# The second tile's matrix scaled and turned in the middle of VectorE's inverse of the first tile

## The chip, the cores and the metric

The kernel runs on one core of one Trainium2 chip. The metric is the time of one execution on the device, in microseconds (us), as the median of several runs.

## The reference

Two parts follow each other. The first is a delta rule over 768 positions, for 4 batches and 8 heads with 48 dimensions; its output, 3072 tokens of 384 values, goes through two feed-forward layers with 2048 hidden values each. Only the first part is touched by the change:

```python
k_n = k / (norm(k) + 1e-06)
for t in range(S):
    y[:, :, t] = einsum('bhd,bhde->bhe', q[:, :, t], state)
    v_old = einsum('bhde,bhd->bhe', state, k_n[:, :, t])
    state = state + beta[t] * einsum('bhd,bhe->bhde', k_n[:, :, t], v[:, :, t] - v_old)
# y: (tokens, 384); then h = x @ w_in, a function of h by element, and g @ w_out, twice
```

## The kernel before, in words

The positions are cut into chunks of C = 32. Four chunks make a tile, so there are T = 6 tiles of 128 positions. Within a chunk the 32 updates depend on each other through a triangular matrix; its inverse turns the 32 steps into matmuls. Each tile has 4 chunks, 4 batches and 8 heads, 128 such matrices of 32 x 32. For the inverse they lie one on each of the 128 partitions, 1024 elements each.

**The inverse** is made by `rounds` (L204 to L218). It starts from the unit matrix and goes through r = 31 down to 1. Round r is a multiply of r x (32 - r) elements into `inv_t` (L214) and a subtract of the same shape into `inv` (L217), each with a wait for the one before: 62 tensor_tensor instructions for one tile, of 31 to 256 elements per partition. All their inputs and outputs are in SBUF. VectorE does tile 0, and GpSimd does tiles 1 to 5, one behind the other. The arguments `first` and `last` of `rounds` give the range of r, and `done` is the count of the engine's own semaphore that has been reached.

**What an inverse needs.** TensorE multiplies keys with keys and queries of a tile (the Gram matrices, `gram_fill`, L374). VectorE then does, for tile j: `weights(j)` (L618 to L625, four short instructions on the norms and beta), four `scale_gram(j, f)` (L641, L642, two multiplies from PSUM each, into `n_mat` and `p_mat`), and two `turn_n(j, ...)` (L659, transposes of half the matrix each into `n_turned`). The second `turn_n` of a tile releases the inverse of that tile on GpSimd. When an inverse is ready, VectorE turns it back with two `turn_x` (L668) into `x_mat`.

**The order of the work** is written out by hand: each engine has one program, and semaphores tie them. VectorE's begins with tile 0's norms, Gram scaling and turning, then the whole inverse of tile 0, then `turn_x(0)`, `residual(0, 0, 0)` (L678), `spread_w(0)` (L650), and then tile 1's `weights`, `scale_gram` and `turn_n`. Behind that comes the loop over tiles and their 8 steps s (4 chunks c, 2 groups g of heads). In a step VectorE does `updates` (L689, from the solve's result), the `residual` of the next step (L678, from the product of keys and state), and `copy_low` (L695, the state). TensorE does in a step: `solve` (L405), a share of the Gram products of the tile two ahead (L374), `q_state` (L418), the next step's `k_state` (L392), `turn_y` (L461), `update` (L432) and `within` (L446). ScalarE copies and scales. The matrix of tile 2 is turned in step 7 of tile 0, that of tile tau + 2 in steps 3 and 4 of tile tau.

Ahead of each tile TensorE runs `keep_warm(BURST)`, 12 matmuls on a zeroed tile whose result nobody reads (L357). For tile 0 it waits for all 62 instructions of VectorE's inverse (`dve_step`), and behind the burst for all eight Gram fills to be scaled (`gram_used`). For the later tiles it waits for the inverse (`inv_ready`). SP issues the loads, each when TensorE or VectorE has done with what lay there; VectorE issues no DMA.

Of the kernel before, what the change touches and what calls it, by code (L numbers as in the profile page):

```python
# [13 lines left out]
C = 32  # L14
# [104 lines left out]
def delta_rule(nc, kq_t, kv_n, beta_n, consts, x1, w1, w, hand):  # L119

    with ExitStack() as ctx:
# [6 lines left out]
        def sem(name):  # L128
            return ctx.enter_context(nc.semaphore(name))
# [47 lines left out]
        pool_step, dve_step = sem("pool_step"), sem("dve_step")  # L177
# [15 lines left out]
        def index(tau, c, g):  # L193
            return NQ * tau + G2 * c + g
# [12 lines left out]
        def rounds(eng, tt, j, own, step, done, first, last):  # L207

            for r in range(first, last, -1):
                shape = [P, r, C - r]  # L210
                prod = inv_t[:, own, 0:r * (C - r)].rearrange("p (i k) -> p i k", i=r)
                if done:
                    eng.wait_ge(step, done)
                tt(prod, n_turned[:, j % 2, r, 0:r].unsqueeze(2).broadcast_to(shape),  # L214
                   inv[:, j % 2, r:r + 1, r:C].broadcast_to(shape), ALU.mult).then_inc(step, 1)
                eng.wait_ge(step, done + 1)
                tt(inv[:, j % 2, 0:r, r:C], inv[:, j % 2, 0:r, r:C], prod, ALU.subtract).then_inc(step, 1)  # L217
                done += 2  # L218
            eng.wait_ge(step, done)
# [364 lines left out]
        def _(dve):  # L584
            dve_tt = nc.vector.tensor_tensor
# [27 lines left out]
            def weights(j):  # L613

                def done(k):
                    dve.wait_ge(norm_step, NORM_STEPS * j + k)
                done(4)
                nc.vector.tensor_scalar(norm[:, j], scratch[:, 3], 0.5, 1e-6, ALU.mult, ALU.add).then_inc(norm_step, 1)  # L618
                done(5)
                nc.vector.reciprocal(scratch[:, 4], norm[:, j]).then_inc(norm_step, 1)  # L620
                done(6)
                dve_tt(scratch[:, 5], scratch[:, 4], beta[:, j], ALU.mult).then_inc(norm_step, 1)
                done(7)
                dve_tt(wgt[:, j], scratch[:, 5], scratch[:, 4], ALU.mult).then_inc(norm_step, 1)
                done(8)  # L625
# [19 lines left out]
            def spread_w(j):  # L645

                if j >= 2:
                    dve.wait_ge(ublk_ready, NQ * (j - 1))
                shape = [P, CG, B]
                dve_tt(w_blk[:, j % 2], wgt[:, j].unsqueeze(2).broadcast_to(shape),  # L650
                       blk_mask[:].unsqueeze(1).broadcast_to(shape), ALU.mult).then_inc(wblk_ready, 1)

            def turn_n(j, a, b):

                dve.wait_ge(gram_used, 4 * j + 4)
                if j >= 3:

                    dve.wait_ge(inv_ready, j - 2)
                nc.vector.transpose(n_turned[:, j % 2, a:b], n_mat[:].rearrange("p n k -> p k n")[:, a:b]  # L659
                                    ).then_inc(n_turned_ready, 1)  # L660

            def turn_x(j, a, b):

                if j:
                    dve.wait_ge(inv_ready, j)
                if j >= 2:
                    dve.wait_ge(hz_done, NQ * (j - 1))
                nc.vector.transpose(x_mat[:, j % 2].rearrange("p n k -> p k n")[:, a:b],  # L668
                                    inv[:, j % 2].rearrange("p i k -> p k i")[:, a:b]).then_inc(x_ready, 1)

            def residual(tau, c, g):
                q = index(tau, c, g)
                dve.wait_ge(nv_ready, q + 1)
                dve.wait_ge(ks_done, q + 1)

                def split(t):
                    return t.rearrange("p (r v) d -> p r v d", r=HALVES)
                dve_tt(split(z[:, g]), split(kv_run[:, c, 1, U * g:U * g + U]),  # L678
                       ks_ps[:, 0:U * D].rearrange("p (v r d) -> p r v d", v=V, r=HALVES), ALU.subtract).then_inc(z_ready, 1)
# [18 lines left out]
            half_k, half_n = C // 2, CG // 2  # L698
# [11 lines left out]
            turn_n(0, half_k, C)  # L710
            dve.wait_ge(inv_blank, 2)
            dve.wait_ge(n_turned_ready, TURNS)
            rounds(dve, dve_tt, 0, 1, dve_step, 0, C - 1, 0)
            turn_x(0, 0, half_k)
            turn_x(0, half_k, C)
            residual(0, 0, 0)
            spread_w(0)
            weights(1)
            for f in range(4):
                scale_gram(1, f)  # L720
            turn_n(1, 0, half_k)
            turn_n(1, half_k, C)
            split = {(T - 2, 2): 0, (T - 2, 6): 1, (T - 1, 2): 2, (T - 1, 6): 3}
            for tau in range(T):
                for s in range(NQ):
# [482 lines left out]
```

## Time and profile before

| | |
|---|---|
| median of 3 runs | 1130.83 us (1129.53 to 1133.27) |
| the profiled execution, own time | 1131.52 us |
| its span | 1129.7 us |
| mean granted TensorE clock | 0.958 |
| TensorE busy | 1026.9 us (91%) |
| VectorE busy | 870.2 us (77%) |
| ScalarE busy | 779.8 us (69%) |
| GpSimd busy | 227.1 us (20%) |

The profile is of one execution of the program. PE is TensorE's matmuls and PEld its weight loads, DVE is VectorE, ACT ScalarE, POOL GpSimd, SP the queue that issues most of the loads. The span begins with the first instruction, and times in the timeline count from there. In a timeline a line gives start, duration, engine, source line, operation, output and inputs, and in brackets the idle time of the engine ahead of it with what ended it; neighbouring instructions of the same kind are put together, with their count behind an x. The delta rule takes the first 292 us of the span, the feed-forward layers the rest. The granted clock is given in shares of TensorE's full 2.4 GHz.

### The profile page before, as it was taken

The numbers are of one execution on the slowest core, as the hardware profiler recorded it, in microseconds if no ns is written. First come the engines' busy times: TensorE is split into PE (matmuls) and PEld (weight loads), VectorE is DVE, ScalarE is ACT, GpSimd is POOL, SyncE is SP. The second block draws the span as 40 slices with busy tenths as digits, with TensorE's granted clock in tenths as the row PEclk, the third lists the DMA queues.
The fourth block names the chain that finished last, engine by engine and source line by source line (L and its number), as shares of the span: only waits on it lengthen the run. The fifth ranks groups of instructions, "written<-read, shape, count | busy, mean of one in ns | idle before, by whom it ended". The sixth has DMA issues, their size and how long they took to land.

```text
span 1129.7 us, 24251 instructions
## 1 busy us (share of the span) xinstructions
PE 1026.9 (91%) x10280; PEld 816.6 (72%) x10280; DVE 870.2 (77%) x948; ACT 779.8 (69%) x991; POOL 227.1 (20%) x380
## 2 busy tenths in 40 slices
PE   4488888888778999999999997999999999999997
PEld 3266666666667888777787876778888888888885
DVE  5966666565388888897887868999787878888885
ACT  1133444465598999989989987986776767676764
POOL 5087888880000010010010000000000000000000
PEclk7578999899989999999999999999999999999999
DMA  7823443323443333435234363430100001010000
GB/s 178 237 60 101 115 130 101 84 77 101 118 91 77 80 91 73 111 63 123 56 67 116 60 168 85 121 112 1 57 1 23 32 0 56 0 56 1 29 1 28
DMA packets 35104, 86.99 MB, mean 77 GB/s; under 512 B 4416, under 2 KB 12096, under 8 KB 35008
## 3 DMA queue, kind: packets, MB, share of 16 engines
q1 hardware_dynamic: 27584, 59.13, 17.3%
q0 software_dynamic: 6912, 25.17, 11.7%
q10 hardware_dynamic: 512, 1.31, 0.5%
q8 instruction: 73, 1.20, 0.4%
q14 instruction: 23, 0.19, 0.1%
HBM read 46.27 MB, written 14.16 MB: 53 GB/s over the span
## 4 chain that ended last, share of the span: by engine, by line
PE 34%; DVE 20%; ACT 12%; issue 6%; DMA 1%; ACTq 0%; DVEq 0%; POOLq 0%
PE o_ps L874 6%; PE o_ps L875 6%; PE o_ps L876 6%; PE h_ps L874 6%; PE h_ps L876 6%; PE h_ps L875 6%; DVE val L1098 5%; DVE den L1055 5%; ACT rec L962 4%; DVE pa L1061 3%; ACT rec L970 2%; DVE val L1082 2%; ACT pa L938 2%; DMA val<-pa 1%; DVE den L1089 1%
## 5 line engine op out<-in xcount | busy, mean ns | idle before, releaser
L874 PE MATMUL o_ps<-g_hi,w_hi_early 128*128 128x512 f32 x288 | 115.6, 401 | 20.8 <-DVE g_lo L1104 15.4
L951 ACT ACTIVATE g_hi<-val 128x1024 fp32r<-128x1024 f32 x96 | 102.0, 1062 | 41.8 <-DVE val L1098 36.1
L865 POOL DMA_DIRECT2D val<-pa x48 | 41.4, 862 | 424.5 <-DVE pa L1061 424.5
L874 PE MATMUL o_ps<-g_hi,w_hi_late 128*128 128x512 f32 x288 | 114.1, 396 | 10.4 <-DVE g_lo L1104 9.9
L1098 DVE SCALAR_TENSOR_TENSOR val<-den,val 128x1024 f32<-128x1024 f32 x96 | 117.4, 1222 | 5.0
L1082 DVE TENSOR_TENSOR val<-val,rec 128x1024 f32<-128x1024 f32 x96 | 117.0, 1219 | 5.5 <-DMA val<-pa 5.5
L1104 DVE SCALAR_TENSOR_TENSOR g_lo<-val,g_hi 128x1024 fp32r<-128x1024 f32 x96 | 117.7, 1226 | 2.0 <-ACT g_hi L951 2.0
L875 PE MATMUL o_ps<-g_lo,w_hi_early 128*128 128x512 f32 x288 | 113.9, 396 | 0.0
L876 PE MATMUL o_ps<-g_hi,w_lo_early 128*128 128x512 f32 x288 | 113.5, 394 | 0.0
L874 PE MATMUL h_ps<-x_hi,w_hi_early 128*128 128x512 f32 x288 | 112.3, 390 | 0.7 <-DVE x_lo L1108 0.4
L875 PE MATMUL o_ps<-g_lo,w_hi_late 128*128 128x512 f32 x288 | 112.9, 392 | 0.0
L876 PE MATMUL o_ps<-g_hi,w_lo_late 128*128 128x512 f32 x288 | 112.9, 392 | 0.0
L876 PE MATMUL h_ps<-x_hi,w_lo_late 128*128 128x512 f32 x288 | 112.1, 389 | 0.0
L876 PE MATMUL h_ps<-x_hi,w_lo_early 128*128 128x512 f32 x288 | 112.1, 389 | 0.0
L875 PE MATMUL h_ps<-x_lo,w_hi_early 128*128 128x512 f32 x288 | 112.1, 389 | 0.0
L874 PE MATMUL h_ps<-x_hi,w_hi_late 128*128 128x512 f32 x288 | 112.1, 389 | 0.0
L875 PE MATMUL h_ps<-x_lo,w_hi_late 128*128 128x512 f32 x288 | 112.1, 389 | 0.0
L970 ACT ACTIVATE rec<-rec 128x1024 f32<-128x1024 f32 x96 | 101.0, 1052 | 1.5
L945 ACT ACTIVATE den<-h_ps 128x1024 f32<-128x1024 f32 x48 | 49.3, 1027 | 66.1 <-PE h_ps L876 66.1
L1089 DVE SCALAR_TENSOR_TENSOR den<-den,rec 128x1024 f32<-128x1024 f32 x48 | 58.8, 1224 | 42.7 <-ACT rec L970 42.7
L214 POOL TENSOR_TENSOR inv_t<-n_turned,inv 128x31 f32<-128x31 f32 (+15 forms) x155 | 78.0, 503 | 55.8 <-DVE n_turned L659 40.0
L217 POOL TENSOR_TENSOR inv<-inv,inv_t 128x31 f32<-128x31 f32 (+15 forms) x155 | 86.4, 558 | 12.1
(114 smaller groups left out, 2175.4 us busy)
## 6 DMA issues: line engine op xcount, KB each, us to landing
val<-pa POOLq DMA_DIRECT2D x48, 512.0 KB, 4.6
w_raw<-w SPq DMA_DIRECT2D x16, 768.0 KB, 5.1
kv_run<-kv_n SPq DMA_DIRECT2D x24, 384.0 KB, 3.8
x_raw<-x_dram SPq DMA_DIRECT2D x12, 768.0 KB, 5.7
kq<-kq_t SPq DMA_DIRECT2D x44, 192.0 KB, 4.0
x_dram<-stage SPq DMA_DIRECT2D x12, 384.0 KB, 4.3
x_dram<-stage SPq DMA_DIRECT2D x6, 768.0 KB, 4.2
out<-stage SPq DMA_DIRECT2D x5, 768.0 KB, 4.1
```

The source lines that it names most:

```text
L214: tt(prod, n_turned[:, j % 2, r, 0:r].unsqueeze(2).broadcast_to(shape), inv[:, j % 2, r:r + 1, r:C].broadcast_to(shape), ALU.mult).then_in ...
L217: tt(inv[:, j % 2, 0:r, r:C], inv[:, j % 2, 0:r, r:C], prod, ALU.subtract).then_inc(step, 1)
L874: nc.tensor.matmul(dst, hi, rhs_hi, start=first, stop=False)
L875: nc.tensor.matmul(dst, hi, rhs_lo, start=False, stop=False)
L876: return nc.tensor.matmul(dst, lo, rhs_hi, start=False, stop=last)
L951: act_fn(g_hi[:, n % 2], val[:, n % 2], ACT.Copy, scale=-1.0).then_inc(g_hi_ready, 1)
L970: act_fn(rec[:, e], rec[:, e], ACT.Exp, scale=-1.0).then_inc(rec_ready, 1)
L1055: dve_stt(den[:, e], sq[:, e], cf[:, 6:7], den[:, e], ALU.mult, ALU.add).then_inc(q_ready, 1)
L1082: dve_tt(val[:, e], val[:, e], rec[:, e], ALU.mult).then_inc(ratio_ready, 1)
L1089: dve_stt(den[:, e], den[:, e], ONE, rec[:, e], ALU.add, ALU.mult).then_inc(unit_ready, 1)
L1098: dve_stt(val[:, e], den[:, e], 2.0, val[:, e], ALU.subtract, ALU.mult).then_inc(g_ready, 1)
L1104: dve_stt(g_lo[:, e], val[:, e], -1.0, g_hi[:, e].bitcast(F32), ALU.mult, ALU.subtract).then_inc(g_lo_ready, 1)
```

## The change

VectorE's inverse of tile 0 is cut into two calls. The first does the rounds r = 31 to 16. Then come tile 1's weights, scaling and turning, which stood behind `spread_w(0)`. The second call does the rounds 15 to 1, with the semaphore's count going on at C = 32. Then follow `turn_x`, `residual` and `spread_w` of tile 0 as before. Nothing else changes.

```diff
@@ -710,16 +710,17 @@
             turn_n(0, half_k, C)
             dve.wait_ge(inv_blank, 2)
             dve.wait_ge(n_turned_ready, TURNS)
-            rounds(dve, dve_tt, 0, 1, dve_step, 0, C - 1, 0)
-            turn_x(0, 0, half_k)
-            turn_x(0, half_k, C)
-            residual(0, 0, 0)
-            spread_w(0)
+            rounds(dve, dve_tt, 0, 1, dve_step, 0, C - 1, C // 2 - 1)
             weights(1)
             for f in range(4):
                 scale_gram(1, f)
             turn_n(1, 0, half_k)
             turn_n(1, half_k, C)
+            rounds(dve, dve_tt, 0, 1, dve_step, C, C // 2 - 1, 0)
+            turn_x(0, 0, half_k)
+            turn_x(0, half_k, C)
+            residual(0, 0, 0)
+            spread_w(0)
             split = {(T - 2, 2): 0, (T - 2, 6): 1, (T - 1, 2): 2, (T - 1, 6): 3}
             for tau in range(T):
                 for s in range(NQ):
```

## Rows read from the trace of the kernel before

**Rows 1.** Waits, 0 to 330 us: engine, line waited for, total us, times, longest us.

```profile
POOL inv_t L214 <- DVE n_turned L659: 40.0, 1, 40.0
```

**Rows 2.** Timeline of GpSimd, inverse of tile 1, 57 to 95 us.

```profile
57.89 0.23 POOL L214 TENSOR_TENSOR inv_t<-n_turned,inv 128x31 f32<-128x31 f32 x1 [39.98 <-DVE n_turned L659]
58.20 0.27 POOL L217 TENSOR_TENSOR inv<-inv,inv_t 128x31 f32<-128x31 f32 x1
...
74.89 0.68 POOL L217 TENSOR_TENSOR inv<-inv,inv_t 128x255 f32<-128x255 f32 x1
...
94.31 0.25 POOL L217 TENSOR_TENSOR inv<-inv,inv_t 128x31 f32<-128x31 f32 x1
```

**Rows 3.** Timeline of TensorE, 35 to 107 us.

```profile
35.97 1.75 PE L374 MATMUL turn_ps<-kq 48*32 48x64 f32 x57 [2.38 <-issue]
...
49.55 4.44 PE L357 MATMUL side_ps<-idle 128*128 128x512 bf16 x12 [11.03 <-DVE inv L217]
55.98 0.54 PE L405 MATMUL hz_ps<-z,x_mat 32*32 32x48 f32 x32 [1.99 <-DVE p_mat L642]
...
58.63 1.55 PE L432 MATMUL st_bank<-u_blk,kv_run 128*64 128x192 f32 x8 [0.67 <-DVE u_blk L689]
...
61.55 1.93 PE L374 MATMUL side_ps<-kq 48*32 48x64 f32 x64
...
101.48 4.08 PE L357 MATMUL side_ps<-idle 128*128 128x512 bf16 x12 [1.12 <-issue]
...
105.97 1.10 PE L374 MATMUL side_ps<-kq 48*32 48x64 f32 x64
```

**Rows 4.** Timeline of VectorE, inverse of tile 1 turned, 101 to 104 us.

```profile
101.95 2.12 DVE L668 STREAM_TRANSPOSE x_mat<-inv 128x512 f32<-128x512 f32 x2
```

**Rows 5.** Timeline of VectorE, 38 to 50 us: start us, us, engine, line, operation.

```profile
38.23 0.42 DVE L214 TENSOR_TENSOR inv_t<-n_turned,inv 128x255 f32<-128x255 f32 x1
...
48.99 0.19 DVE L214 TENSOR_TENSOR inv_t<-n_turned,inv 128x31 f32<-128x31 f32 x1
49.22 0.19 DVE L217 TENSOR_TENSOR inv<-inv,inv_t 128x31 f32<-128x31 f32 x1
```

**Rows 6.** Timeline of VectorE, 51 to 107 us.

```profile
51.87 0.20 DVE L618 TENSOR_SCALAR norm<-scratch 128x32 f32<-128x32 f32 x1
...
52.94 0.42 DVE L641 TENSOR_TENSOR n_mat<-st_bank,wgt 128x256 f32<-128x256 f32 x1
...
55.72 2.02 DVE L659 STREAM_TRANSPOSE n_turned<-n_mat 128x512 f32<-128x512 f32 x2
57.66 0.92 DVE L689 TENSOR_TENSOR u_blk<-hz_ps,w_blk 128x768 f32<-128x768 f32 x1
...
65.05 0.35 DVE L678 TENSOR_TENSOR z<-kv_run,ks_ps 128x192 f32<-128x192 f32 x1 [1.75 <-PE ks_ps L392]
...
82.36 0.35 DVE L678 TENSOR_TENSOR z<-kv_run,ks_ps 128x192 f32<-128x192 f32 x1 [4.27 <-PE ks_ps L392]
...
106.10 0.96 DVE L689 TENSOR_TENSOR u_blk<-hz_ps,w_blk 128x768 f32<-128x768 f32 x1 [2.03 <-PE hz_ps L405]
```

**Rows 7.** Timelines of GpSimd and VectorE where both work in SBUF, 80 to 240 us.

```profile
80.07 0.60 POOL L214 TENSOR_TENSOR inv_t<-n_turned,inv 128x247 f32<-128x247 f32 x1
...
129.57 0.59 POOL L217 TENSOR_TENSOR inv<-inv,inv_t 128x192 f32<-128x192 f32 x1
...
129.59 0.62 DVE L611 TENSOR_TENSOR scratch<-scratch,root 128x32 f32<-128x32 f32 x1
...
237.22 2.50 POOL L214 TENSOR_TENSOR inv_t<-n_turned,inv 128x247 f32<-128x247 f32 x1
...
237.51 1.74 DVE L100 TENSOR_TENSOR w_lo_early<-w_raw,w_hi_early 128x1536 fp32r<-128x1536 f32 x1
```

**Rows 8.** Stretches: window, us, busy us (instructions) by engine, granted clock, DMA share, GB/s.

```profile
64.00:66.00 2.00, 2.00 (x30) 1.45 (x22) 0.91 (x3) 0.00 (x0) 1.76 (x4) 0.50 0.31 86
106.00:108.00 2.00, 1.54 (x82) 1.24 (x81) 0.96 (x1) 0.00 (x0) 1.76 (x4) 1.00 0.00 0
```

## The prediction

> **What bounds the kernel now.** The page comes first: the change lies in the first part of the span, where TensorE, VectorE and GpSimd all work and where the GpSimd engine has nearly all of its busy time. The chain of waits is no help here, because it reaches back only to the feed-forward layers. So I read the waits of the stage and then the timeline of each engine.
>
> The waits up to 330 us have one large row for the inverse on GpSimd: it stands idle for 40.0 us until the second tile's turned matrix comes from VectorE [rows 1]. That idle time is what the change shortens. What matters is whether anybody waits at the other end, and no row of that view has an engine waiting for a finished inverse. For tile 1 the timeline shows it directly. GpSimd starts at 57.89 and ends at 94.56 [rows 2]. TensorE starts its burst for tile 1 at 101.48 [rows 3], and VectorE turns the inverse at 101.95 [rows 4]. The inverse lies ready 6.9 us before its first user. The inverses of the later tiles can't start earlier through this change, since tile 2's matrix is turned only in the last step of tile 0.
>
> What does set the start of tile 0 is VectorE. It works without a pause from the first inverse to the first update: rounds 15 to 1 of the inverse from 38.23 to 49.41 [rows 5], turning it, the residual and the spread weights to 51.87, tile 1's weights to 52.94, scaling to 55.72, turning to 57.66. There the first update starts [rows 6]. The matmuls that it needs are done at 56.5 [rows 3]. From then on the tile is a chain between TensorE and VectorE with little slack: each later start of the first update moves everything behind it.
>
> **The work that moves.** Weights, scaling and turning for tile 1 take 57.66 - 51.87 = 5.79 us. They go from behind the spread weights into the middle of the inverse. Nothing is added or removed, and no DMA is issued by VectorE. Tile 1's products are in PSUM at 37.72 [rows 3], and the scaling would start near 38.2 + 1.1 = 39.3, so no wait comes in; if those products came later, VectorE would wait there with the rest of its inverse behind it. I cost this at nothing. SP's loads wait on TensorE and for nothing in this block, and they are issued before it ends; they move with the chain.
>
> Work moved within one engine ahead of the same first update would cost nothing if VectorE set both times. It doesn't quite. TensorE starts a burst of 12 warming matmuls when the inverse is done: 49.55, 0.14 us behind it, for 4.44 us [rows 3]. The first solve is queued behind the burst. Today the burst and the solve are covered by the 5.79 us that now leave. For tile 1, which has no such cover, the first update starts 106.10 - 101.48 = 4.62 us after the burst starts, with a burst of 4.08; with 4.44 it is 4.98, so 5.12 us after the inverse's end [rows 3, 6]. Today it is 57.66 - 49.41 = 8.25. The end of the inverse moves by 5.79, the tail shrinks by 3.13: **+2.66 us**.
>
> **The two engines at once.** This is the largest and the least certain term. Today VectorE has the inverse of tile 0 alone. After the change GpSimd starts its rounds at the moment when VectorE goes on with its rounds 15 to 1, and both are tensor_tensor instructions with two inputs in SBUF. The trace shows what happens between such instructions. VectorE's L100, 1.74 us long, stretches a GpSimd multiply of 247 elements from 0.60 to 2.50; the GpSimd instruction ends 0.47 us after VectorE's. The other way round, L611 starts at 129.59 beside a GpSimd instruction that started at 129.57, and takes 0.62 in place of some 0.19; it ends 0.05 after GpSimd's [rows 7]; the 0.19 is that of 31 elements [rows 5]. So they don't overlap: each waits for the one that came first, and has the first 0.14 of its own duration (0.19 less 0.05; 0.60 less 0.47) behind it by then.
>
> Bounds. Below: nothing, if VectorE always gets in first, as L100 did; a gain has no row, as VectorE alone is the fastest case shown. Above: a whole GpSimd instruction in front of each of the 30. Those 30 that run first take 75.57 - 57.89 = 17.68 us, 0.59 each with a pause of 0.08 (58.12 to 58.20), so 0.51 without it [rows 2]; 30 x 0.51 = 15.3 us. What I take: both engines work in pairs that wait for their own last result, with short pauses of 0.04 on VectorE and 0.08 on GpSimd, so whoever is finished finds the other one waiting, and they alternate. GpSimd then holds 0.51 - 0.14 = 0.37 us per turn, of which VectorE hides its own pause and start, 0.04 + 0.14 = 0.18 [rows 5]. Each of the 30 grows by 0.19: **+5.7 us**. It is nearest to the L611 row, which is the one where both started together. The rounds on VectorE then take 11.2 + 5.7 = 16.9 us.
>
> The Trainium skill, "SBUF — State Buffer", section "Who interferes with whom", speaks against this change: a VectorE instruction with two SBUF inputs contends with a GpSimd one that reads SBUF, and the first to issue has the port for its whole instruction while the other fully blocks. On who blocks, the trace agrees (2.50 in place of 0.60); on the length, the rows show 0.14 less than the whole. By the rule read strictly the sum would be +14.6 us, as in the third rival.
>
> GpSimd loses a similar share, but starts some 13.5 us earlier and ends before 90; its cover of 6.9 us grows.
>
> **TensorE's clock.** Behind the burst TensorE now idles from 53.99 to 55.98, and the steps that follow run at the lower clock: the granted clock reads 0.50 in 64:66, which is 1.2 GHz. It reads 1.00 (2.4 GHz) in 106:108, in tile 1, where the solve follows the burst at once [rows 3, 8]. After the change the solve follows the burst at once here too, so I expect the full clock in tile 0's first two steps. The first state update takes 1.55 us at the low clock; the Gram fill behind the second solve takes 1.93 for 64 matmuls, against 1.10 at the full clock. At that ratio the update saves 0.7. Of VectorE's wait of 1.75 us for the keys' product at 65.05 [rows 6] some 1.5 goes. **-2.2 us**. Bounds: 0 if the clock stays low, and -2.4 if the 1.75 goes whole.
>
> **The sum.** 2.66 + 5.7 - 2.2 = +6.2 us. The profiled execution took 1131.52 us with a span of 1129.7, so 1137.7 for one like it. It lies 0.7 above the median of 1130.83, which I take as the base: 1137.0.
>
> **The rivals.**
> 1. The clock stays at 1.2 GHz in the first steps, because TensorE has idled some 12 us longer ahead of the burst. For it: the clock rose only late in today's burst. Against it: tile 1's. 2.66 + 5.7 = +8.4, 1139.2. Chance 0.18.
> 2. VectorE hardly waits, because its next instruction takes the port before GpSimd's: as with L100, where GpSimd had started 0.29 earlier and still waited. Against it: L611 waited, and L100 followed an earlier instruction without waiting for its result, which the rounds never do. With 0 to 1 us for that term the sum is +0.5 to +1.5, about 1131.8: no difference. Chance 0.14.
> 3. A blocked instruction starts anew: 30 x (0.51 - 0.04) = 14.1 for that term, +14.6 in all, 1145.4. Against it: both rows of an end 0.14 early. Chance 0.05. The rule of the Trainium skill's SBUF page, read strictly, is this case.
> 4. Faster: TensorE stands still in the key product of tile 0's fifth step, and VectorE waits 4.27 us for it at 82.36 [rows 6]. The profile gives no releaser but "issue". If the new timing filled that gap (instructions fetched while TensorE waits longer for the inverse), the sum is 2.66 - 2.2 - 4.3 = -3.8 with nothing for the port, 1127.0. It is over 0.3% faster only if the port costs under 0.4 us; with my 5.7 it ends at +1.9. Against it: TensorE already idles 11 us ahead of the burst today. Chance 0.08.
>
> That the change does nothing is no case: the order of VectorE's queue differs, and GpSimd's start follows it.
>
> **How the numbers follow.** My forecast (+3.5 to +8, its port term between 3 and 7.5) has 0.55. The range leaves out rivals 3 and 4 and reaches from rival 2 to rival 1 with some 2 us of port wait above it: 1131.3 to 1141.3. A measurement of this kernel can tell 0.3% from no change, 3.4 us. Slower by more than that: the forecast and rivals 1 and 3, 0.78. Within: rival 2, and the part of rival 4 where the port costs over 0.4 us, 0.15. Faster: the rest of rival 4, 0.07.
>
> **What would show it.** GpSimd's first instruction for tile 1 near 44.2 us. VectorE's rounds 15 to 1 from 44.0 over some 17 us with durations near 0.6 in place of 0.37, and GpSimd's beside them longer by a little. The burst near 61, the solve right behind it, the first update near 66.3, and a granted clock of 1.00 behind it. Tile 1's burst some 6 us later than 101.5, and still no wait for an inverse. Rounds of 11 to 12 us beside a busy GpSimd would put me wrong towards no change; a wait of the burst of tile 1 for an inverse would put my reading of what bounds the kernel wrong.

## The result and the profile after

The changed kernel is slower. Its median is 1139.23 us over 8 runs (1136.69 to 1145.86), against 1132.94 for the kernel before over 8 runs. The ratio is 1.0077 with a 95% interval of 1.0056 to 1.0098, which is 8.7 us (6.3 to 11.1). The two medians by themselves lie 6.3 us apart, at the lower end of that. Timed once more (e11, below) the ratio is 1.0067, 1.0042 to 1.0092, 7.6 us, and there the medians lie 9.7 us apart. So the size is 8 us, known to some 2 us. The forecast was +6.2 us, or 0.55%. The direction and the mechanism of the loss were right and the size came out too small: 0.55% lies just under the first interval and inside the second.

In the profiled execution, 1138.97 us, the span grew from 1129.7 to 1137.2. VectorE's timeline of the changed kernel, to set beside [rows 5, 6, 4]:

```profile
43.98 0.39 DVE L214 TENSOR_TENSOR inv_t<-n_turned,inv 128x255 f32<-128x255 f32 x1
44.40 0.42 DVE L217 TENSOR_TENSOR inv<-inv,inv_t 128x255 f32<-128x255 f32 x1
...
50.44 0.54 DVE L217 TENSOR_TENSOR inv<-inv,inv_t 128x207 f32<-128x207 f32 x1
...
60.37 0.69 DVE L214 TENSOR_TENSOR inv_t<-n_turned,inv 128x31 f32<-128x31 f32 x1
61.09 0.19 DVE L217 TENSOR_TENSOR inv<-inv,inv_t 128x31 f32<-128x31 f32 x1
61.32 2.14 DVE L668 STREAM_TRANSPOSE x_mat<-inv 128x512 f32<-128x512 f32 x2
...
67.57 0.96 DVE L689 TENSOR_TENSOR u_blk<-hz_ps,w_blk 128x768 f32<-128x768 f32 x1 [3.38 <-PE hz_ps L405]
...
72.50 0.33 DVE L678 TENSOR_TENSOR z<-kv_run,ks_ps 128x192 f32<-128x192 f32 x1
...
108.25 2.11 DVE L668 STREAM_TRANSPOSE x_mat<-inv 128x512 f32<-128x512 f32 x2
```

Rounds 15 to 1 start at 43.98 and end at 61.28. They take 17.30 us where they took 11.18. The last multiply, 31 elements, takes 0.69 in place of 0.19. GpSimd's timeline beside it, which answers to [rows 2]:

```profile
44.21 0.25 POOL L214 TENSOR_TENSOR inv_t<-n_turned,inv 128x31 f32<-128x31 f32 x1 [26.29 <-DVE n_turned L659]
...
50.26 0.50 POOL L214 TENSOR_TENSOR inv_t<-n_turned,inv 128x175 f32<-128x175 f32 x1
...
60.34 0.67 POOL L217 TENSOR_TENSOR inv<-inv,inv_t 128x252 f32<-128x252 f32 x1
...
81.42 0.25 POOL L217 TENSOR_TENSOR inv<-inv,inv_t 128x31 f32<-128x31 f32 x1
```

GpSimd starts 13.7 us earlier than before and is done at 81.67 instead of 94.56. Nobody picks this inverse up earlier: VectorE turns it at 108.25, now 26.6 us after its end. Set the two timelines side by side at one point. GpSimd's multiply of 175 elements starts at 50.26 and ends at 50.76. VectorE's subtract of 207 elements starts at 50.44 and ends at 50.98, 0.22 after GpSimd's; alone it takes 0.37, and less the 0.14 that lies behind it by then that is 0.23. They alternate, as forecast.

But the price is not the same for every instruction. VectorE's first six lose nothing (0.42 for 252 elements, as alone), and the loser there is GpSimd, whose multiply of 60 elements takes 0.39 in place of 0.28. VectorE's last multiply loses 0.50, beside a GpSimd instruction of 252 elements that takes the 0.67 it takes undisturbed. By these rows the engine with the shorter instruction waits. The forecast's 0.19 for each is close to the average, 6.1 / 30 = 0.20.

TensorE's timeline, which answers to [rows 3]:

```profile
61.43 5.28 PE L357 MATMUL side_ps<-idle 128*128 128x512 bf16 x12 [22.31 <-DVE inv L217]
66.64 0.86 PE L405 MATMUL hz_ps<-z,x_mat 32*32 32x48 f32 x32
...
68.58 0.87 PE L432 MATMUL st_bank<-u_blk,kv_run 128*64 128x192 f32 x8 [0.29 <-DVE u_blk L689]
...
70.19 1.10 PE L374 MATMUL side_ps<-kq 48*32 48x64 f32 x64
...
107.77 4.44 PE L357 MATMUL side_ps<-idle 128*128 128x512 bf16 x12 [2.30 <-issue]
```

The burst takes 5.28 us in place of 4.44, all of it at the low clock, and the solve follows it at once. The first update starts at 67.57 against 57.66, 9.9 us later. Behind it the clock is full for some 10 us, as the windows show (columns as in [rows 8]); in 78:80 it reads 0.50 again.

```profile
60.00:62.00 2.00, 0.57 (x2) 0.28 (x3) 1.90 (x4) 0.00 (x0) 1.76 (x4) 0.50 0.00 0
64.00:66.00 2.00, 2.00 (x6) 0.68 (x5) 0.18 (x1) 0.00 (x0) 1.76 (x4) 0.50 0.00 0
70.00:72.00 2.00, 2.00 (x121) 1.71 (x108) 2.00 (x3) 1.46 (x6) 1.76 (x4) 1.00 0.04 8
```

The state update takes 0.87 in place of 1.55 and the Gram fill 1.10 in place of 1.93. The residual of the next step no longer waits: it starts at 72.50 and before at 65.05, 7.4 us apart. So two steps at the full clock have given back 2.5 us. Up to the turning of tile 1 at 108.25 the loss has shrunk to 6.3 us, the forecast's number. But the timed runs say 8.7 and 7.6. Which term was too small was the question of the experiments.

One wait stands in this profile that the kernel before doesn't have, and it is for an inverse. The end of tile 5's inverse on GpSimd and its turning on VectorE, first before, then after:

```profile
255.32 0.25 POOL L217 TENSOR_TENSOR inv<-inv,inv_t 128x31 f32<-128x31 f32 x1
257.76 2.12 DVE L668 STREAM_TRANSPOSE x_mat<-inv 128x512 f32<-128x512 f32 x2
```

```profile
262.10 0.25 POOL L217 TENSOR_TENSOR inv<-inv,inv_t 128x31 f32<-128x31 f32 x1
262.43 2.14 DVE L668 STREAM_TRANSPOSE x_mat<-inv 128x512 f32<-128x512 f32 x2 [1.69 <-POOLq L345]
```

GpSimd does the inverses of tiles 2 to 5 back to back, in 155.8 us before and 156.3 after. They start when tile 2's matrix is turned, in the last step of tile 0, and the change makes that later, 106.03 in place of 99.73. Before, the last of them was ready 2.2 us ahead of its user; now VectorE waits 1.7 us for it and TensorE's burst 2.1.

### The profile page after: what moved, and what is told of

Its sections match the earlier page's. It is cut to its first block, busy times and chain, and to the rows that moved or that the text cites. A ratio compares the mean times of both kernels' runs of the same rounds, so it can differ in the third digit from the quotient of the medians.

```text
span 1137.2 us, 24252 instructions
## 1 busy us (share of the span) xinstructions
PE 1023.9 (90%) x10280; PEld 813.5 (72%) x10280; DVE 875.1 (77%) x948; ACT 780.3 (69%) x991; POOL 228.5 (20%) x380
## 4 chain that ended last, share of the span: by engine, by line
PE 35%; DVE 19%; ACT 12%; issue 6%; DMA 1%; ACTq 0%; DVEq 0%; POOLq 0%
PE o_ps L875 6%; PE o_ps L877 6%; PE o_ps L876 6%; PE h_ps L877 6%; PE h_ps L875 6%; PE h_ps L876 6%; DVE val L1099 5%; DVE den L1056 5%; ACT rec L963 4%; DVE pa L1062 3%; ACT rec L971 2%; DVE val L1083 2%; ACT pa L939 2%; DMA val<-pa 1%; DVE den L1090 1%
## 5 line engine op out<-in xcount | busy, mean ns | idle before, releaser
L217 POOL TENSOR_TENSOR inv<-inv,inv_t 128x31 f32<-128x31 f32 (+15 forms) x155 | 88.8, 573 | 12.2
```

## The experiments

All ratios are to runs of the kernel before, taken beside the experiment. Line numbers shift by a few where lines were added.

**e1: GpSimd waits for VectorE.**

```diff
                 pool.wait_ge(n_turned_ready, TURNS * (j + 1))
+                if j == 1:
+                    pool.wait_ge(dve_step, STEPS)
```

> The changed kernel, but GpSimd's inverse of tile 1 waits until VectorE has finished its whole inverse of tile 0, so the two never run at once. Theory (the shared access of two SBUF inputs costs the 6 us): rounds 15 to 1 take 11.2 us again in place of 17.3, the inverse ends near 55.2, the first update starts near 61.5 with a burst of 5.3 us, tile 1's inverse is turned near 102.2 (before 101.95, changed kernel 108.25), and the time is that of the kernel before within 0.3%. Rival (the rounds are slow because of where they stand, or the loss is in TensorE's burst and clock): the rounds keep some 17 us, tile 1's turning stays near 108, and the time stays 0.5 to 0.8% above before.

Measured: 1.0008 (0.9991 to 1.0026). VectorE's timeline:

```profile
44.97 0.39 DVE L214 TENSOR_TENSOR inv_t<-n_turned,inv 128x255 f32<-128x255 f32 x1
...
55.92 0.19 DVE L217 TENSOR_TENSOR inv<-inv,inv_t 128x31 f32<-128x31 f32 x1
...
61.98 0.96 DVE L691 TENSOR_TENSOR u_blk<-hz_ps,w_blk 128x768 f32<-128x768 f32 x1 [3.29 <-PE hz_ps L407]
```

The 30 instructions take 11.14 us again, and the first update is 5.6 us earlier than in the changed kernel, or 6.6 when the 1.0 us is taken off by which this execution's first round came late. No loss in time is left that the interval would show. The same instructions at the same place in the queue are slow only while GpSimd works. The rival falls.

**e4: the block further back**, so that 10 instructions and not 30 run beside GpSimd.

```diff
-            rounds(dve, dve_tt, 0, 1, dve_step, 0, C - 1, C // 2 - 1)
+            rounds(dve, dve_tt, 0, 1, dve_step, 0, C - 1, 5)
...
-            rounds(dve, dve_tt, 0, 1, dve_step, C, C // 2 - 1, 0)
+            rounds(dve, dve_tt, 0, 1, dve_step, 2 * (C - 6), 5, 0)
```

> The changed kernel with the block put in after round 6 and not after round 16, so that only 10 of VectorE's instructions run beside GpSimd's. Theory (each pair costs GpSimd's hold less what VectorE hides): the last 10 take 2.8 us alone and some 3.5 to 4.5 with GpSimd's short first instructions beside them, the inverse ends near 56.5, the first update near 62.5, tile 1's turning near 103, time some 1 to 2 us above before. Rival (a fixed cost of cutting the inverse, however many instructions follow): rounds 5 to 1 lose as much as 15 to 1 did, 6 us, and the time stays that of the changed kernel.

Measured: 1.0024 (1.0005 to 1.0043). First and last of the 10:

```profile
52.34 0.26 DVE L214 TENSOR_TENSOR inv_t<-n_turned,inv 128x135 f32<-128x135 f32 x1
...
55.30 0.43 DVE L214 TENSOR_TENSOR inv_t<-n_turned,inv 128x31 f32<-128x31 f32 x1
55.77 0.19 DVE L217 TENSOR_TENSOR inv<-inv,inv_t 128x31 f32<-128x31 f32 x1
```

The time is 2.7 us above the kernel before, a little more than the 1 to 2 expected. The 10 take 3.62 us against 2.79 alone, so 0.8 lost. In the changed kernel the same 10 take 6.48, because GpSimd is by then at its long instructions. So the cost is set by what stands on the other engine, and not by a fixed price of cutting the inverse.

**e9 and e10: what on GpSimd's side blocks.** In both GpSimd waits as in e1, and does 24 other instructions of 256 elements meanwhile, in a spare tile.

```diff
+                    for i in range(24):
+                        nc.gpsimd.memset(spare[:, 1], 0.0).then_inc(filled, 1)              # e9
+                        nc.gpsimd.tensor_copy(spare[:, 1], spare[:, 0]).then_inc(filled, 1) # e10
+                        pool.wait_ge(filled, i + 2)
```

> GpSimd's inverse of tile 1 waits for VectorE's of tile 0 as in e1, but meanwhile GpSimd does 24 memsets of 256 elements into a spare tile: it writes SBUF and reads nothing. If it is the read of SBUF that the two engines contend for: rounds 15 to 1 take 11.2 us as alone. Rival (any SBUF work of GpSimd beside a two-input instruction blocks): they take 14 us or more.

> As e9, but the 24 instructions are copies of 256 elements from one spare tile to another: one SBUF input, one output. If GpSimd's read is what contends: rounds 15 to 1 take clearly more than 11.2 us, 11.2 plus each copy's duration less 0.14 and less the 0.18 that VectorE hides, so some 2 to 5 us more by how long a copy takes. Rival (it takes two inputs on GpSimd's side as well): 11.2 us.

Each was profiled once and not timed. The memsets, with one of VectorE's subtracts beside them:

```profile
44.72 8.79 POOL L350 MEMSET spare<- 128x256 f32 x24 [26.23 <-DVE n_turned L668]
```

and on VectorE:

```profile
44.94 0.42 DVE L219 TENSOR_TENSOR inv<-inv,inv_t 128x255 f32<-128x255 f32 x1
```

The copies:

```profile
44.75 11.74 POOL L350 COPY spare<-spare 128x256 f32<-128x256 f32 x24 [26.24 <-DVE n_turned L668]
```

and on VectorE:

```profile
44.94 0.50 DVE L219 TENSOR_TENSOR inv<-inv,inv_t 128x255 f32<-128x255 f32 x1
```

Beside the memsets the 30 instructions take 11.12 us, as alone. By itself this shows little: with memsets of 0.31 us the prediction's formula leaves VectorE nothing to wait, 0.31 - 0.14 - 0.18. GpSimd's side decides. A memset of 256 elements at the start of the execution, long before VectorE's inverse, takes the same 0.31 as the 24 do on average:

```profile
0.75 0.31 POOL L331 MEMSET idle<- 128x256 f32 x1 [0.29 <-POOLq L1210]
```

And one memset follows another every 8.79 / 24 = 0.37 us, beside VectorE's instructions that at first come every 0.46, so the two don't take turns. Beside the copies the 30 take 13.32 us, and the subtract of 255 elements 0.50 in place of 0.42. One SBUF input on GpSimd's side is enough, and its writes alone do nothing. A copy takes 0.43 us on average, in this same run. The formula gives 0.43 - 0.14 - 0.18 = 0.11 for each, 2.6 us for 24; measured are 2.1.

The Trainium skill says the same of who blocks whom ("SBUF — State Buffer", "Who interferes with whom": a VectorE instruction with two SBUF inputs contends with a GpSimd one that reads SBUF, not with one that only writes). These two runs agree. The same section of the Trainium skill tells of blocking for the whole instruction where VectorE is in one of its 2-port modes. Read strictly for these instructions too, as the prediction did, it would have put 14.1 us on the rounds; the changed kernel shows 6.1.

**e2: the burst released 4 instructions before the inverse's end.**

```diff
-            pe.wait_ge(dve_step, STEPS)
+            pe.wait_ge(dve_step, STEPS - 4)
```

> The changed kernel, with TensorE's warming burst released 4 instructions before the end of VectorE's inverse. Theory (the burst of 5.3 us is what the first solve waits for once the 5.8 us of cover are gone): burst from 58.9 to 64.2, the first update near 64.6 in place of 67.57, so 3 us earlier, and the clock still full after it; the time 2 to 3 us below the changed kernel. Rival (the solve waits for z and the update for VectorE's own work): first update within 0.5 us of 67.57 and no change of the time.

Measured: 1.0042 (1.0019 to 1.0064). TensorE's burst and VectorE's first update:

```profile
60.03 5.28 PE L357 MATMUL side_ps<-idle 128*128 128x512 bf16 x12 [20.65 <-DVE inv L217]
```

and on VectorE:

```profile
65.97 0.96 DVE L689 TENSOR_TENSOR u_blk<-hz_ps,w_blk 128x768 f32<-128x768 f32 x1 [0.83 <-PE hz_ps L405]
```

The inverse ends at 62.24 here, so the update starts 3.7 us behind it in place of 6.3. Of the tail, 2.6 us was the burst alone. The time moves the same way by 3 to 4 us, though the intervals overlap.

**e8: no burst ahead of tile 0 in the changed kernel** (12 matmuls that feed nothing are left out).

```diff
-            pe.wait_ge(dve_step, STEPS)
-            by_event()
-            keep_warm(BURST)
             pe.wait_ge(gram_used, 8)
```

> The changed kernel without the warming burst ahead of tile 0 (it computes nothing that is used). Theory (the burst only delays the first solve, and its clock is worth less than its 5.3 us): first solve when z is ready, first update 3.0 to 3.5 us behind the inverse's end in place of 6.3, the first steps at 0.50 and some 2 us longer, tile 1's turning 1 to 2 us earlier than in the changed kernel, time 0 to 2 us below it. Rival (the full clock of the first steps is worth more than the burst): tile 1's turning later than in the changed kernel and the time above it.

Measured: 1.0050 (1.0028 to 1.0072). The solve and the first update:

```profile
64.62 0.86 PE L405 MATMUL hz_ps<-z,x_mat 32*32 32x48 f32 x32 [25.66 <-DVE z L675]
65.41 0.87 PE L418 MATMUL y_bank<-state,kq 128*32 128x96 f32 x16
```

and on VectorE:

```profile
65.55 0.96 DVE L686 TENSOR_TENSOR u_blk<-hz_ps,w_blk 128x768 f32<-128x768 f32 x1 [0.41 <-PE hz_ps L405]
```

The update starts 3.3 us behind the inverse's end at 62.24, as expected, and the first matmuls run at the low clock (0.86 and 0.87). Tile 1's turning is at 109.43 (this execution's start lies 1 us later), not earlier as expected, while the time is no worse than the changed kernel's. The intervals don't separate it from the changed kernel or from e2.

**e7: how much the second inverse has to spare.** The kernel before, with GpSimd's tile 1 held back.

```diff
                 pool.wait_ge(n_turned_ready, TURNS * (j + 1))
+                if j == 1:
+                    pool.wait_ge(ublk_ready, 3)
```

> The kernel before, but GpSimd's inverse of tile 1 waits until the third update of tile 0 is done, near 70 us, 12 us later than today. Theory (its end has 6.9 us to spare today, which is why starting it earlier gains nothing): it ends near 106.8, tile 1's burst and turning wait for it and come 5 to 6 us later than 101.5 to 102, and the time rises by 4 to 6 us. Rival (the inverse is not on the path at all, or the slack is larger): turning of tile 1 stays within 1 us and the time is the same.

Measured: 1.0038 (1.0019 to 1.0058), 4.3 us. First and last instruction of that inverse, then the waits between 60 and 110 us (who waited for whom, total us, times, longest us):

```profile
67.14 0.23 POOL L214 TENSOR_TENSOR inv_t<-n_turned,inv 128x31 f32<-128x31 f32 x1 [49.24 <-DVE u_blk L691]
...
103.88 0.25 POOL L217 TENSOR_TENSOR inv<-inv,inv_t 128x31 f32<-128x31 f32 x1
```

```profile
PE side_ps L359 <- POOLq L347: 7.6, 1, 7.6
...
DVE x_mat L670 <- POOLq L347: 5.2, 1, 5.2
```

The third update was done sooner than expected, so GpSimd started at 67.14 and not near 70, 9.3 us late. The inverse ends at 104.13, and both users wait for it. That is the wait which the kernel before does not have. The turning itself is 2.3 us later than before and not the expected 5 to 6. At tile 5 VectorE waits for GpSimd once more, 3.0 us, because the later inverses stand in line behind this one. So the slack of tile 1 is real and is used up before 9.3 us, and an earlier start had nothing to gain there.

**e5, e6, e11: the two kernels once more, unchanged**, e11 timed.

> The kernel before, unchanged, profiled once more. It asks how far one profile speaks for the others. If the clock term of the prediction is a property of the kernel: inverse end to first update 8.25 us, first update to tile 1's turning 44.3 within 0.5, clock 0.50 in the first steps again. If it is chance of one execution: the stretch from first update to tile 1's turning lies 1 us or more off 44.3, or x_lo of the first layer to the first g_lo lies 1 us or more off 21.0.

> The changed kernel, unchanged, profiled once more. Property of the kernel: rounds 15 to 1 in 17.3 us, burst 5.3 us, inverse end to first update 6.3, first update to tile 1's turning 40.7 within 0.5. Chance: any of them 1 us or more off.

> The changed kernel once more, timed, to size the total against the repeatable shift of the first update (+9.8 us) . If the clock gain after it is worth the forecast 2.2 us: 0.5 to 0.8% above before, 6 to 9 us. If it is worth nothing on average: 0.8 to 0.95%. Its profile gives the stretches behind the first update a third time.

e11: 1.0067 (1.0042 to 1.0092). That lies where it was expected with the clock gain, and its interval takes in most of what was expected without. e5 is the important one. VectorE's first update, the turning of tile 1 and the start of the feed-forward part, in e5 and then the last of these in the kernel before:

```profile
57.66 0.92 DVE L689 TENSOR_TENSOR u_blk<-hz_ps,w_blk 128x768 f32<-128x768 f32 x1
...
103.47 2.14 DVE L668 STREAM_TRANSPOSE x_mat<-inv 128x512 f32<-128x512 f32 x2
...
304.39 1.76 DVE L1108 TENSOR_TENSOR x_lo<-x_raw,x_hi 128x1536 fp32r<-128x1536 f32 x1 [1.32 <-ACT x_hi L974]
```

```profile
295.46 1.76 DVE L1108 TENSOR_TENSOR x_lo<-x_raw,x_hi 128x1536 fp32r<-128x1536 f32 x1 [1.32 <-ACT x_hi L974]
```

It is the same program. The first update starts at 57.66 in both, to the hundredth. Tile 1's turning is 1.5 us later in e5, and the feed-forward part starts 8.9 us later; the time of that execution is 1141.39 us against 1131.52. Up to the end of the first inverse VectorE's rows repeat within 0.1 us, apart from the first round of the inverse, which starts at 26.1 in 9 of the 17 profiles of all kernels and 0.6 to 1.4 us later in the others. TensorE's burst doesn't repeat: 4.44 us in the first profile, 5.22 in e5, covered in both. Behind the first update one execution says little: the stretch from there to tile 1's turning is 45.8 us in e5 against 44.3, and 41.6 and 42.5 in e6 and e11 against 40.7. The three profiles of the changed kernel (first, e6, e11) agree in the rounds (17.30, 17.29, 17.28) and have tile 1's turning within 0.8 us (108.25, 109.07, 108.67). The tail from the inverse's end to the first update takes 6.3, 6.2 and 4.9 us, by how early in the burst the clock rises.

**e3, e12, e13, e14: the clock of the first steps by itself.** All are the kernel before, and their first update stays 8.2 to 8.3 us behind the inverse's end. In e3 and e13 the burst waits for the turned inverse, so that the solve follows at once. In e12 and e14 there is no burst ahead of tile 0 (as in e8).

```diff
-            pe.wait_ge(dve_step, STEPS)
+            pe.wait_ge(x_ready, TURNS)        # e3, e13
```

> The kernel before, with the warming burst held until VectorE has turned the inverse (2 us later), so that the solve follows it at once. Theory (the pause between burst and solve is what costs the clock in tile 0's first steps, worth some 2 us): granted clock 1.00 from about 56 on, first update near 57.7 as before or up to 0.6 later, tile 1's inverse turned at 99.5 to 100.5 in place of 101.95, time 1.5 to 2.5 us below the kernel before. Rival (the clock falls in the first steps whatever stands ahead of them): clock 0.50 again in 60:66 and no gain.

> The kernel before without the burst ahead of tile 0, which is covered there and costs nothing itself. If the clock of tile 0's first steps is worth 2 us or more: solve at 55.98 at the low clock, first update at 58.0, low clock for longer, time 1 to 4 us above before. Rival (the clock there is worth nothing that lasts): time within 0.15% of before.

> The kernel of e3 once more (before, burst held until the inverse is turned, full clock in tile 0's first steps). If the clock gain reaches the end: 0.15 to 0.25% below before, and below e14 by 0.2% or more. If it is given back before the end: within 0.1% of before and of e14.

> The kernel of e12 once more (before, no burst ahead of tile 0, low clock in its first step). If the clock gain reaches the end: at before or above it, and 0.2% or more above e13. If it is given back: within 0.1% of e13.

| | what stands ahead of the first solve | ratio | interval |
|---|---|---|---|
| e3 | burst, then the solve at once | 1.0007 | 0.9987 to 1.0026 |
| e13 | the same | 1.0002 | 0.9976 to 1.0028 |
| e12 | no burst | 0.9990 | 0.9967 to 1.0014 |
| e14 | no burst | 0.9983 | 0.9960 to 1.0007 |

The clock does what was expected. In e3's window 60:62 it is 1.00, and tile 1 is turned at 100.58 though VectorE's inverse of tile 0 ended 1.0 us later than in the kernel before, 2.4 us earlier by that count:

```profile
60.00:62.00 2.00, 2.00 (x116) 1.57 (x114) 1.45 (x2) 1.43 (x6) 1.69 (x5) 1.00 0.00 0
```

and VectorE's first update and tile 1's turning:

```profile
58.66 0.92 DVE L689 TENSOR_TENSOR u_blk<-hz_ps,w_blk 128x768 f32<-128x768 f32 x1
...
100.58 2.16 DVE L668 STREAM_TRANSPOSE x_mat<-inv 128x512 f32<-128x512 f32 x2
```

But the time doesn't follow: no gain in e3 and e13, and no loss in e12 and e14, which lean the other way. e14 was to lie above e13 or within 0.1% of it, and its ratio is 0.2% below. The expected gain of 2.2 us would be a ratio of 0.9981. That lies outside e3's interval and inside e13's. The profiles show how far the gain is steady. The table gives, in us, how late each point is against the first profile of the kernel before, less what the execution's first round was already late:

| | first update | residual of the next step | tile 1 turned | feed-forward part starts |
|---|---|---|---|---|
| kernel before again (e5) | 0.0 | 0.0 | 1.5 | 8.9 |
| changed kernel: first, e6, e11 | 9.9, 9.8, 8.5 | 7.4, 7.3, 6.1 | 6.3, 7.1, 6.7 | 5.3, 5.8, 13.1 |
| e3, e13 (full clock at once) | 0.0, 0.0 | -2.5, -2.5 | -2.4, -3.1 | -1.4, -0.2 |
| e12, e14 (no burst) | 0.0, -0.1 | -1.6, -0.1 | 0.9, -2.9 | 5.9, -1.8 |

Up to the next step's residual the full clock gives 2.5 us in all five profiles that have it there. At tile 1's turning e14, without a burst, is as early as e3 and e13, and one kernel's executions already differ by 1.5 us. So the gain is real in the first two steps and can't be followed beyond them. The windows of e13, and behind them those of e12, show one place where it can go:

```profile
58.00:100.00 42.00, 32.66 (x1123) 24.71 (x1125) 28.25 (x58) 18.08 (x58) 35.69 (x72) 0.96 0.35 105
100.00:200.00 100.00, 85.15 (x2707) 62.94 (x2707) 57.13 (x106) 40.54 (x130) 87.11 (x164) 0.91 0.37 102
```

```profile
58.00:100.00 42.00, 36.31 (x1090) 27.67 (x1084) 24.55 (x48) 16.35 (x52) 32.89 (x64) 0.78 0.29 78
100.00:200.00 100.00, 85.10 (x2754) 61.04 (x2754) 61.88 (x117) 42.33 (x136) 86.42 (x165) 0.95 0.40 114
```

Up to 100 us the granted clock is 0.96 in e13 and 0.78 in e12; from 100 to 200 it is 0.91 and 0.95. In e3 the two are 0.92 and 0.93, in e14 0.85 and 0.98. So in these four, where the first stretch has more of the clock, the second has somewhat less. But e5, with 0.78 in the first stretch as in e12, has 0.90 in the second. This is an observation and no cause.

**e15: both costs taken out**, GpSimd's wait of e1 and the burst 8 instructions early.

```diff
+                if j == 1:
+                    pool.wait_ge(dve_step, STEPS)
...
-            pe.wait_ge(dve_step, STEPS)
+            pe.wait_ge(dve_step, STEPS - 8)
```

> The changed kernel with GpSimd waiting for VectorE's whole inverse as in e1, and the burst released 8 instructions ahead of its end. Port and burst are both taken out: inverse end near 55.3 to 56.1, first update 3.0 to 3.5 us behind it, near 59, 1 to 1.5 us behind before's 57.66, full clock after it. Time within 0.15% of before by either view of the clock; above 0.3% would say that something else in the change costs.

Measured: 0.9988 (0.9967 to 1.0008). The end of the inverse is at 56.45, and the first update 3.0 us behind it:

```profile
56.48 2.11 DVE L670 STREAM_TRANSPOSE x_mat<-inv 128x512 f32<-128x512 f32 x2
...
59.45 0.96 DVE L691 TENSOR_TENSOR u_blk<-hz_ps,w_blk 128x768 f32<-128x768 f32 x1 [0.46 <-PE hz_ps L407]
```

With the port and the burst out, the change costs nothing that can be measured. It also brings nothing: no version tried is faster than the kernel before by more than its interval.

**What the clock is worth, from all runs together.** If nothing happened behind the first update, a kernel would be slower by as much as its first update is late. The table sets the two side by side. The lateness is the profile's, less what the execution's first rounds were already late.

| | first update later, us | time longer, us | difference |
|---|---|---|---|
| changed kernel (first, e11) | 9.9, 8.5 | 8.7, 7.6 | -1.2, -0.9 |
| e1 | 3.3 | 0.9 | -2.4 |
| e2 | 7.3 | 4.8 | -2.5 |
| e4 | 4.4 | 2.7 | -1.7 |
| e8 | 6.9 | 5.7 | -1.2 |
| e15 | 0.4 | -1.4 | -1.8 |
| e3, e13 (full clock at once) | 0.0, 0.0 | 0.8, 0.2 | +0.8, +0.2 |
| e12, e14 (no burst) | 0.0, 0.0 | -1.1, -1.9 | -1.1, -1.9 |

Each time has an interval of about 2 us to either side, and the lateness is of one execution, so no single row decides. The kernels with the changed order all lie 0.9 to 2.5 us on the side of a gain, e8 with its low clock at the start among them. e3 and e13, where only the clock differs from the kernel before, keep none. So there may be a small gain behind the first update, but that the clock of the first steps makes it is not shown, and the cleanest test speaks against it. This stays open.

## Why the prediction was right, and where it was wrong

- **What bounds the kernel.** Right for the inverse that the change starts earlier: nobody waits for tile 1's, before or after, and e7 had to delay it by 9.3 us to make a wait. But the prediction asked only whether the later inverses could start earlier. The inverses of tiles 2 to 5 start later through the change, and tile 5's had only 2.2 us to spare. In the first profile of the changed kernel it is waited for, 1.7 us; in e6 and e11 it lies ready 0.8 and 2.5 us before its user. What this costs in the timed runs is not shown.
- **The work that moves, +2.66.** Right in kind, short in size. The inverse's end moved by 5.8 and the port term, as forecast. The tail behind it was taken as 5.12 us, from a burst of 4.44. The three profiles give 6.3, 6.2 and 4.9, in two of them because the burst ran at the low clock throughout (5.28). On average that is 0.7 us short.
- **The two engines at once, +5.7.** Right in kind: 17.30 - 11.18 = 6.1, the same in three executions, 0.4 us short. That the size came so close is in part luck. The formula takes the same 0.19 for each of the 30, and the trace shows 0 for the first six and 0.50 for the last multiply. There GpSimd's instruction takes 0.67, for which the formula gives 0.67 - 0.14 - 0.18 = 0.35: that instruction starts when VectorE's has ended (60.34, after 60.33), so it hasn't waited, and the 0.14 that the formula takes off for it isn't there: 0.67 - 0.14 - 0.04 = 0.49. Too much for the early ones and too little for the late ones came out nearly even. Rival 2 (VectorE hardly waits) and rival 3 (a blocked instruction starts anew, the strict rule) are both out. e1, e9 and e10 show the cause.
- **TensorE's clock, -2.2. This is the step that failed**, as a term of the sum. The clock came, and where the term was read it came in full size: 2.5 us by the residual of the next step, in all three profiles. But the term was taken to stand at the end of the kernel, and nothing in the prediction showed that it would. Where it was tried by itself (e3 and e13) nothing of it reached the time. The first update is 9.4 us late on average of the three profiles and the two timed ratios give 8.2, so in the place of -2.2 the runs leave -1.2, with some 2 us to either side. That is a difference of two averages and no measurement of the clock. The other two terms, which the profiles do measure, were short by 0.7 and 0.4. With them the sum is 2.66 + 0.7 + 6.1 = 9.5 us, and 8.3 with the -1.2; with the forecast's -2.2 it would be 7.3. Why the gain of the first steps doesn't last is open.
- **Rival 1** named 8.4 us, close to the time, but its reason, a clock that stays low in the first steps, did not occur. The clock stayed low through the burst alone, which is part of the 0.7 us above. That its number fits is luck.
- **Rival 4** (the standstill at 82.36 filled in) came in part. That wait shrank from 4.27 to 2.07 us in the first profile, and the step gives back 2.2, 1.9 and 0.7 us in the three. The sum had nothing for it. But in e3 and e14, whose order is that of the kernel before, the same step gives back 0.9 and 1.2 us, so this need not come from the change, and no timed run separates it.
- **The base.** The sum was set on a median of three runs, 1130.83 us. More runs of the same kernel gave 1132.94, and beside the experiments 1133.5 to 1135.2. On such a base +8.7 us ends at 1141.7, beyond the range's upper end of 1141.3, while the measured median of 1139.23 lies inside it. The range was worked out for the change's terms alone, and took no part for the base.

## What to carry to other kernels

- Work that is moved to release another engine earlier pays only if somebody waits for that engine's result: look for the wait at the far end before the one at the near end. One wait of 40 us stood in the view, and filling 13.7 us of it was worth nothing. Then look at every later piece of work on that engine: here the last one, four inverses on, had 2.2 us to spare, and the change moved it back.
- Two elementwise chains that both read SBUF, one on VectorE with two inputs and one on GpSimd, cost each other time when they run side by side. Price it pair by pair: in this trace the engine with the shorter instruction of the two waited, and an average over all pairs hid losses from 0 to 0.50 us.
- Trust a single profile for a stretch only as far as a second one repeats it. Here that was to 0.1 us up to the end of the first inverse, and to 1.5 us at tile 1 and 9 us at the feed-forward part behind it.

## What the runs showed of the hardware that was not expected

- GpSimd's memsets cost nothing beside VectorE's two-input instructions (11.12 us for 30, and 0.31 for a memset beside them as alone), and a copy with a single SBUF input does (13.32).
- The cost is one-sided. GpSimd's 62 instructions took 37.5 us in the changed kernel against 36.7 before, while VectorE's 30 lost 6.1. GpSimd lost at its short first ones (0.39 in place of 0.28 for 60 elements), VectorE at its short last ones (0.69 in place of 0.19 for 31).
- One program's executions differ by 10 us in 1130 with VectorE's first update at 57.66 in both. The difference arises between the first update and the start of the feed-forward part, where the granted clock of the window 58 to 290 us varies from one execution to the next. Why, is open.
